# Attention with top-k, then two feed-forward blocks: a step's order remade on four engines

## The reference

```python
scores = scale * np.matmul(q, k.transpose(0, 1, 3, 2))
kth = np.partition(scores, -top_k, axis=-1)[..., -top_k:-top_k + 1]
scores = np.where(scores >= kth, scores, -1000000000.0)
attn = np.exp(scores - np.max(scores, axis=-1, keepdims=True))
x = heads_side_by_side(np.matmul(attn / (attn.sum(-1, keepdims=True) + 1e-09), v))
h = x @ w_in
g = np.maximum(h, 0.0) + alpha * np.minimum(h, 0.0)
y = g @ w_out
out = (y @ w_a) * (y @ w_b) @ w_o
```

## Time and profile before

| | |
|---|---|
| median of 3 runs | 655.65 us (655.42 to 656.97) |
| profiled execution | 659.29 us, of it the span 657.5 us |
| PE busy | 607.9 us, 92% |
| VectorE (DVE) busy | 425.1 us, 65% |
| ScalarE (ACT) busy | 355.5 us, 54% |
| GpSimd (POOL) busy | 291.3 us, 44% |
| busy tenths of VectorE in 40 slices | 4999999999899999999999006364331222112111 |
| busy tenths of PE in 40 slices | 5577799998999999899898989989999999999997 |

### The profile page before, as it was taken

How to read it: one execution, slowest core, us unless ns; L and a number is a source line. 1 busy time by engine, 2 the same in 40 slices (tenths; PEclk the granted TensorE clock), 3 DMA queues, 4 the chain that set the end, 5 groups by cost and what they waited for, 6 DMA issues and landing times.

```text
span 657.5 us, 10894 instructions
## 1 busy us (share of the span) xinstructions
PE 607.9 (92%) x4192; PEld 507.8 (77%) x4192; DVE 425.1 (65%) x847; ACT 355.5 (54%) x642; POOL 291.3 (44%) x285
## 2 busy tenths in 40 slices
PE   5577799998999999899898989989999999999997
PEld 3355576676787878777776867879999999999996
DVE  4999999999899999999999006364331222112111
ACT  3499987877777777776667536353322122121111
POOL 0266779899988898877878650000000000000000
PEclk9889989999999999999999989989999999999999
DMA  7889962223113333342240430840011000010001
GB/s 258 318 295 368 353 224 62 78 67 85 58 42 96 125 110 106 103 129 93 79 127 21 157 121 17 283 164 1 0 49 49 0 1 1 0 49 1 0 1 48
DMA packets 30914, 68.06 MB, mean 104 GB/s; under 512 B 2704, under 2 KB 7312, under 8 KB 30736
## 3 DMA queue, kind: packets, MB, share of 16 engines
q1 hardware_dynamic: 30864, 67.38, 30.9%
HBM read 53.22 MB, written 14.16 MB: 102 GB/s over the span
## 4 chain that ended last, share of the span: by engine, by line
PE 50%; DVE 34%; POOL 8%; issue 4%; ACT 2%; DMA 2%; SPq 0%; ACTq 0%; POOLq 0%
DVE top L700 18%; DVE work L708 16%; PE ps L962 7%; PE ps L960 7%; PE ps L961 7%; PE ps L974 4%; PE ps L975 4%; PE ps L973 4%; PE ps L860 2%; PE ps L862 2%; PE ps L861 2%; POOL p_sb L432 2%; POOL wout_lo L419 2%; PE ps L892 2%; PE ps L895 2%
## 5 line engine op out<-in xcount | busy, mean ns | idle before, releaser
L700 DVE MAX8 top<-work 128x8 f32<-128x576 f32 x216 | 152.4, 749 | 0.0
L432 POOL TENSOR_TENSOR p_sb<-s_sb,p_sb 128x576 f32<-128x576 f32 x72 | 101.8, 1426 | 18.6 <-ACT p_sb L534 18.6
L708 DVE MATCH_REPLACE8 work<-top,work 128x576 f32<-128x576 f32 x144 | 106.1, 746 | 0.0
L753 DVE TENSOR_TENSOR ab<-ps,a_sb 128x384 f32<-128x384 f32 x36 | 20.1, 558 | 132.3 <-PE ps L962 132.3
L960 PE MATMUL ps<-y_parts,wab 128*128 128x384 f32 x288 | 97.3, 338 | 0.0
L962 PE MATMUL ps<-y_parts,wab 128*128 128x384 f32 x288 | 96.7, 336 | 0.0
L961 PE MATMUL ps<-y_parts,wab 128*128 128x384 f32 x288 | 96.4, 335 | 0.0
L540 ACT ACTIVATE p_sb<-p_sb,neg_max 128x576 f32<-128x576 f32 x72 | 56.4, 784 | 50.0 <-POOL p_sb L432 49.9
L860 PE MATMUL ps<-win_hi,xT_parts 128*128 128x512 f32 x144 | 61.2, 425 | 11.1 <-POOL xT_parts L449 8.4
L534 ACT ACTIVATE p_sb<-s_sb,kth_big 128x576 f32<-128x576 f32 x72 | 55.3, 787 | 11.0 <-POOL neg_max L427 11.0
L669 ACT ACTIVATE ab_hi<-ab 128x384 fp32r<-128x384 f32 x36 | 18.9, 524 | 77.2 <-DVE ab L753 77.2
(11 more groups left out here) (88 smaller groups left out, 1350.5 us busy)
## 6 DMA issues: line engine op xcount, KB each, us to landing
v_sb<-in_v SPq DMA_DIRECT2D x36, 320.0 KB, 2.9
s_dram<-keep_sb SPq DMA_DIRECT2D x16, 576.0 KB, 4.8
s_sb<-s_dram SPq DMA_DIRECT2D x16, 576.0 KB, 3.7
k_sb<-in_kT SPq DMA_DIRECT2D x24, 288.0 KB, 4.1
win_raw<-in_w_in SPq DMA_DIRECT2D x4, 1024.0 KB, 7.4
wout_raw<-in_w_out SPq DMA_DIRECT2D x4, 1024.0 KB, 9.0
wab_raw<-in_w_a SPq DMA_DIRECT2D x8, 384.0 KB, 3.9
...
```

The costliest lines, as they stand in the source:

```text
L432: nc.gpsimd.tensor_tensor(p_sb[:, chain.par, c, :], s_sb[:, chain.slot, c, :], p_sb[:, chain.par, c, :], ALU.subtract).then_inc(masked, 1)
L700: largest = nc.vector.max(top32[:, pair.par, c, 8 * r:8 * r + 8], work[:, c, :] if r else s_sb[:, pair.slot, c, :])
L708: nc.vector.match_replace(work[:, c, :], top32[:, pair.par, c, 8 * r:8 * r + 8], work[:, c, :] if r else s_sb[:, pair.slot, c, :], -3.0e38)\
```

## The change

A pair is turned and multiplied by v one step earlier: the first part of pair i + 1 is turned in the step in which it is masked, `times_v` of pair i runs in step i. The x turn and the first block follow one step earlier (FIRST_UP 4, last step 35). h itself is turned (`copy_of_h`, `turn_h`), and max(h, 0), max(-h, 0), slope and sum come after the turn, with features along partitions: alpha is then one column per 128 features, loaded as 8 KB in place of 1 MB, and the transposed result needs one more step to its high part (`hi_of_g`). The keys of batch 0 are loaded once into SBUF. The split tile is the second, not the first. Four slots, not two, hold kept scores; they lie where w_out is loaded later. The first scores wait for the query and half the keys, and are made head by head. The orders of all four engines within a step, and in the tail, are rewritten. The rest of the tail goes on in the pattern shown.

```diff
-SLOTS = 2
+SLOTS = 4
 FIRST_STEP = -2
-LAST_STEP = N_PAIRS
-FIRST_UP = PAIRS + 1
+LAST_STEP = N_PAIRS - 1
+FIRST_UP = 4
 LAST_UP = LAST_STEP - FIRST_UP
-AHEAD = {-2: [0, 1, 2], -1: [3, 4, 5], 0: [6, 7], 1: [8, 9], 2: [10, 11], 3: [12, 13], 4: [14, 15]}
-W_IN_AT = {-1: [0], 0: [1], 1: [2], 2: [3], 3: [4], 4: [5], 5: [6], 6: [7]}
+AHEAD = {-2: [0, 1], -1: [2, 3, 4], 0: [5, 6, 7], 1: [8, 9, 10], 2: [11, 12, 13], 3: [14, 15]}
+W_IN_AT = {-1: [0], 0: [1], 1: [2], 2: [3], 3: [4, 5], 4: [6], 5: [7]}
 W_OUT_AT = {7: [0], 8: [1], 9: [2, 3], 10: [4], 11: [5, 6], 12: [7]}
-LOADS_AT = {-1: ["in1"], 0: ["in2"], 1: ["in3"], 2: ["out0"], 3: ["out1"], 4: ["alpha", "out2"], 5: ["out3"]}
+LOADS_AT = {-2: ["in0"], -1: ["in1"], 0: ["in2"], 1: ["alpha", "in3"], 4: ["out0"], 5: ["out1"], 6: ["out2"], 7: ["out3"]}
+DVE_FROM = LAST_UP - 1
+SPLIT = 1
...
+        keep_sb = at("keep_sb", [P, SLOTS, 2 * S], reg_wout_lo)
+        qa_sb = at("qa_sb", [P, KEPT // PAIRS, PAIRS, P], reg_wout_lo + 4 * SLOTS * 2 * S)
+
+        k_sb, reg_att = new("k_sb", [P, PAIRS, S])
         q_sb, _ = new("q_sb", [P, KV, P])
...
         def x_turn(i):
 
-            tile, rest = divmod(i - FIRST_UP, QUADS)
-            return tile if rest == 0 and 0 <= tile and i <= LAST_STEP else None
+            tile, rest = divmod(i - PAIRS + 1, PAIRS)
+            return tile if rest == 0 and 0 <= tile < TILES else None
...
-            for p in range(KV):
-                load_kq(pair(p))
-                load_k1(p)
-            load_qa(WHOLE + 1)
-            for p in range(KV, PAIRS):
-                load_k1(p)
-            load_first_block("in0")
+            load_q(pair(0))
+            sp.dma_start(k_sb[0:D, 0, :], kT[0, 0, 0:D]).then_inc(k0_half_in, 16)
+            sp.dma_start(k_sb[D:P, 0, :], kT[0, 0, D:P]).then_inc(k0_in[0], 16)
+            load_q(pair(1))
+            load_k0(1)
+            load_qa(0)
+            load_k1(0)
+            load_k1(1)
+            load_k0(2)
+            load_k1(2)
+            load_k0(3)
+            load_k1(3)
+            load_qa(1)
             for p in range(2):
                 sp.wait_ge(scored, p + 1)
-                load_kq(pair(KV + p))
-            load_qa(WHOLE + 2)
-            for i in range(FIRST_STEP, LAST_STEP):
+                load_q(pair(KV + p))
+            for i in range(FIRST_STEP, LAST_STEP + 1):
                 if i == FIRST_STEP + 1:
                     load_v(pair(0))
                     load_v(pair(1))
...
                 if i > FIRST_STEP and i + 5 < DIRECT:
                     sp.wait_ge(scored, i + 4)
-                    load_kq(pair(i + 5))
-                if i in (0, 1):
-                    sp.wait_ge(ahead, PAIRS * (i + 1))
-                    load_qa(WHOLE + 3 + i)
+                    load_q(pair(i + 5))
+                if i in (-1, 0):
+                    load_qa(i + 3)
                 for n in AHEAD.get(i, []):
                     save_scores(n)
+                if i == min(n for n in LOADS_AT if LOADS_AT[n][0] == "out0"):
+                    for slot in range(SLOTS):
+                        sp.wait_ge(kept_saved[slot], 16 * KEPT // SLOTS)
...
             def slope_and_sum(seq):
                 q = seq % QUADS
-                pool.wait_ge(u_free, up_use(seq) + 1)
-                nc.gpsimd.tensor_tensor(neg[:, :], neg[:, :], alpha_sb[:, q * 512:(q + 1) * 512], ALU.mult)\
-                  .then_inc(slope_done, 1)
+                pool.wait_ge(halves_done, seq + 1)
+                if 0 < seq < QUADS + 1:
+                    pool.wait_ge(down_done, seq)
+                sides = neg[:, :].rearrange("p (f n) -> p f n", f=QUADS)
+                slopes = alpha_sb[:, q * QUADS:(q + 1) * QUADS].unsqueeze(2).to_broadcast([P, QUADS, P])
+                nc.gpsimd.tensor_tensor(sides, sides, slopes, ALU.mult).then_inc(slope_done, 1)
                 pool.wait_ge(slope_done, seq + 1)
-                nc.gpsimd.tensor_tensor(pos[:, :], pos[:, :], neg[:, :], ALU.subtract).then_inc(sum_done, 1)
+                if seq > QUADS:
+                    pool.wait_ge(ghi_done, seq - QUADS)
+                nc.gpsimd.tensor_tensor(gT[:, :, :].rearrange("p f n -> p (f n)"), pos[:, :], neg[:, :], ALU.subtract)\
+                  .then_inc(sum_done, 1)
 
             def lo_of_g(seq):
-                pool.wait_ge(ghi_done, seq + 1)
+                pool.wait_ge(ghi_done, seq + 1 - QUADS)
                 nc.gpsimd.tensor_tensor(g_lo, gT[:, :, :], g_hi.bitcast(f32), ALU.subtract).then_inc(glo_done, 1)
 
             def step(i):
-                chain, output, finished = pair(i + 1), pair(i), pair(i - 1)
+                chain, output = pair(i + 1), pair(i)
                 if chain is not None:
                     bound(chain)
+                if x_turn(i - 1) is not None:
+                    lo_of_x(x_turn(i - 1))
                 if output is not None and output.hp == PAIRS - 1:
                     denominator(output)
-                if turning(i) is not None:
-                    slope_and_sum(turning(i))
+                if rounded(i) is not None and QUADS <= rounded(i) < DVE_FROM:
+                    lo_of_g(rounded(i))
                 if chain is not None:
                     mask(chain, 0)
-                if x_turn(i) is not None:
-                    lo_of_x(x_turn(i))
-                if finished is not None and finished.hp == PAIRS - 1:
-                    normalise(finished)
-                if chain is not None:
-                    mask(chain, 1)
                 for c in W_IN_AT.get(i - 1, []):
                     lo_of_w_in(c)
                 for c in W_OUT_AT.get(i - 1, []):
                     lo_of_w_out(c)
-                if turning(i) is not None and turning(i) >= QUADS:
-                    lo_of_g(turning(i))
+                if chain is not None:
+                    mask(chain, 1)
+                if output is not None and output.hp == PAIRS - 1:
+                    normalise(output)
+                if turning(i) is not None and turning(i) < DVE_FROM:
+                    slope_and_sum(turning(i))
 
             for i in range(FIRST_STEP, LAST_STEP + 1):
                 if i == FIRST_UP + 1:
                     pool.wait_ge(alpha_in, 16)
                 step(i)
-            slope_and_sum(LAST_UP)
...
+                if c == 0:
+                    act.wait_ge(pv_done, (SPLIT + 1) * PAIRS)
+                    act.wait_ge(kept, KEPT)
...
-                at = SC[0] + c * S
-                act.wait_ge(scored, 1)
+                at = SC[1 - c] + c * S
+                if c == 0:
+                    act.wait_ge(half_scored, 1)
+                else:
...
-            def halves_of_h(seq):
+            def copy_of_h(seq):
                 act.wait_ge(u_full, up_use(seq) + 1)
                 if seq:
                     act.wait_ge(gt_full, seq)
-                else:
-                    for slot in range(SLOTS):
-                        act.wait_ge(kept_saved[slot], 16 * KEPT // SLOTS)
-                nc.scalar.activation(pos[:, :], ps[:, U, :], ACT.Relu)
-                nc.scalar.activation(neg[:, :], ps[:, U, :], ACT.Relu, scale=-1.0).then_inc(u_free, 1)
-
-            def parts_of_g(seq):
-                src = ps[:, GT, :].rearrange("p (f n) -> p f n", f=QUADS)
+                nc.scalar.activation(h_sb[:, :], ps[:, U, :], ACT.Copy).then_inc(u_free, 1)
+
+            def halves_of_h(seq):
                 act.wait_ge(gt_full, seq + 1)
                 if seq:
+                    act.wait_ge(sum_done, seq)
+                nc.scalar.activation(pos[:, :], ps[:, GT, :], ACT.Relu)
+                nc.scalar.activation(neg[:, :], ps[:, GT, :], ACT.Relu, scale=-1.0).then_inc(halves_done, 1)
+
+            def hi_of_g(seq):
+                act.wait_ge(sum_done, seq + 1)
+                if seq > QUADS:
                     act.wait_ge(down_done, seq)
-                if seq < QUADS:
-                    nc.scalar.activation(gT[:, :, :], src, ACT.Copy).then_inc(ghi_done, 1)
-                else:
-                    nc.scalar.activation(g_hi, src, ACT.Copy)
-                    nc.scalar.activation(gT[:, :, :], src, ACT.Copy).then_inc(ghi_done, 1)
+                nc.scalar.activation(g_hi, gT[:, :, :], ACT.Copy).then_inc(ghi_done, 1)
...
-                score, chain, output, finished = direct(i), pair(i + 1), pair(i), pair(i - 1)
+                score, chain, output = direct(i), pair(i + 1), pair(i)
                 ahead_now = AHEAD.get(i, [])
-                if turning(i) is not None:
-                    halves_of_h(turning(i))
-                if output is not None:
-                    evict_turned(output, 0)
+                if x_turn(i - 1) is not None:
+                    evict_x_turn(x_turn(i - 1))
+                if rounded(i) is not None and rounded(i) >= QUADS:
+                    hi_of_g(rounded(i))
                 if chain is not None:
                     relu(chain, 0)
-                if x_turn(i) is not None:
```

(114 more changed lines are left out.)

136 lines of the change are left out of this document (87 added, 49 removed).

## The result

The changed kernel takes 660.4 us in the median (659.65 to 665.5) against 655.5 for the kernel before on the same chip: ratio 1.0087, 95% interval 1.0064 to 1.0111. It is 4.8 us slower, where 4.5 us faster was forecast, and lies above the range.

What follows compares the result with a forecast made beforehand. VectorE's ranking at 9.66 us a pair, then PE's tail, bound the kernel. Span 657.5 - 1.1 (start) + 3.8 (middle) - 7.2 (tail) = 653.0; the change of -4.5 put on the median 655.65 gave 651.2 us, range 644.5 to 656.5.

Steps and rivals of the forecast that it cites:

- the edits costed at nothing: Side edits priced at nothing, among them four keep slots, alpha's load, k loads and ScalarE's work per quad.
- The walk through the middle: Ranking from step 6: GpSimd's same-step waits for down and heavy steps make VectorE wait 6.95 against 3.14, 3.8 us lost.
- Start: First scores, made head by head after smaller loads, let VectorE start ranking earlier: gain 1.1 us (0.3 to 1.9).
- Slope: GpSimd's slope with alpha as a broadcast operand takes 1046 ns, not 1289: 0.24 us off each quad.
- Tail: End of ranking to second block: 52.4 us against 60.3, 7.9 shorter, of which 7.2 was counted.
- The two waits of 1.6: Tail: PE idles 1.6 us before down(32) and again before down(33), as one up does not hide a quad's chain.
- (d): Rival: waits for lo_of_x at each tile's first up bring PE to 1.2 GHz, 2.3 us each, five times: 662.7; chance 0.10.
- (b): Rival: the middle is worse, slope at 1289 (+1.2) and a wait before up(4) slowing PE (+2.3): 654.7; chance 0.09.
- (c): Rival: the tail's two waits of 1.6 us slow PE's clock, some 1.5 us each: 654.2; chance 0.05.

Runs made afterwards that it cites:

- g2: e8 with saved scores spread 4, 3, 3, 2, 2, 2 and, in steps with two saves, both through the second score buffer; 657.7 us.
- e2: Changed kernel with a second place for g, so GpSimd's slope_and_sum in steps 7 to 9 waits for the down of the step before; 661.0 us.
- g1: Changed kernel with w_out's parts in earlier steps: two each in steps 7 and 8, then one a step; 656.4 us.
- g6: Kernel before the change with w_out's parts in steps 7: 0 and 1, 8: 2 and 3, then one a step; 653.4 us.
- e7: Changed kernel with w_a and w_b parts moved behind copy_of_h in the tail, lo_of_w2 behind lo_of_g, tile 7's y evicted earlier; 660.7 us.
- e6: Changed kernel with the second turn of a pair ahead of the direct score in PE's step, in all steps; 666.2 us.
- e8: Changed kernel with the second turn ahead of the direct score in steps -2 to 3 only; 658.7 us.
- e10: Changed kernel with GpSimd's low parts of w_in and w_out behind the second mask of the step, not between the masks; 664.3 us.
- e1: Changed kernel with the 16 saved scores spread 4, 3, 3, 2, 2, 2 over steps -2 to 3 in place of 2, 3, 3, 3, 3, 2; 666.4 us.
- e13: Changed kernel with work left out: GpSimd makes w_out's low part for 64 of 512 columns, PE uses the high part instead; 657.3 us.
- e3: Changed kernel with VectorE's reciprocal in the last of the four rounds instead of the second; 664.7 us.
- e4: Changed kernel with the edits of e1, e2 and e3 together; 665.9 us.
- b0: A second profiled execution of the kernel before, with no edit; 656.18 us.
- b5: Kernel before with only the change's spread of saved scores, 2, 3, 3, 3, 3, 2 in steps -2 to 3; 658.7 us.

## Why the prediction was wrong

**The step that failed** is the sentence on four keep slots under the edits costed at nothing: "Three scores ahead in a step instead of two make ScalarE's early steps about 9.9 us against 9.66, and the copy has more than 6 us to spare." It counted ScalarE's busy time and put the effect at nothing. What sets the early step is a ring over two engines: ScalarE's saved copy at the end of its step, PE's direct score that needs its buffer, PE's turn behind the score, ScalarE's copy of the turned pair, relu, and the next copies. ScalarE's copies of pairs 5, 6 and 7 and PE's wait before the first x turn in the changed kernel:

```profile
52.49 1.12 ACT L537 ACTIVATE s_sb<-ps 128x1152 f32<-128x1152 f32 x1
...
62.71 1.12 ACT L537 ACTIVATE s_sb<-ps 128x1152 f32<-128x1152 f32 x1
...
76.05 1.12 ACT L537 ACTIVATE s_sb<-ps 128x1152 f32<-128x1152 f32 x1
```

```profile
70.17 0.44 PE L916 MATMUL ps<-ident,x_sb 128*128 128x128 f32 x1 [3.86 <-ACT keep_sb L554]
```

A step takes 10.2 us at best in this ring, and the one with the first x turn 13.3 (76.05 - 62.71): `turn_x(0)` waits for the last save, the score of pair 7 stands behind it, and PE runs at a granted 0.50 from 70 to 75. Of the room of 6.7 us 2.7 were left before the heavy steps began, and pair 7 waited 2.38 us besides. g2 takes the ring away and the copy comes at 79.9: ranking ends 4.3 us earlier, at 365.9. The step with the first x turn stays 13.4 us long even there (copies at 58.40 and 71.75), with the same wait for the last save; no run takes that wait away. The span missed its forecast by 8.1 us (3.6 slower for 4.5 faster), and 4.3 of them are this ring.

**The walk through the middle** had the right increments on a wrong start. GpSimd's timeline of the changed kernel, two slopes of the light steps and then the bounds of steps 10 to 13:

```profile
99.01 1.04 POOL L476 TENSOR_TENSOR neg<-neg,alpha_sb 128x512 f32<-128x512 f32 x1 [2.11 <-PE ps L957]
...
122.82 1.04 POOL L476 TENSOR_TENSOR neg<-neg,alpha_sb 128x512 f32<-128x512 f32 x1 [3.47 <-PE ps L957]
...
136.35 0.19 POOL L442 TENSOR_SCALAR kth_big<-top 128x2 f32<-128x2 f32 x1
...
148.23 0.19 POOL L442 TENSOR_SCALAR kth_big<-top 128x2 f32<-128x2 f32 x1
...
158.88 0.19 POOL L442 TENSOR_SCALAR kth_big<-top 128x2 f32<-128x2 f32 x1
...
171.75 0.19 POOL L442 TENSOR_SCALAR kth_big<-top 128x2 f32<-128x2 f32 x1
```

The steps from 136.35 take 11.9, 10.7 and 12.9 us; 11.6, 10.6 and 12.8 were forecast. But the first is at 136.35, forecast 129.9, and all are 6.4 to 6.9 late. With the ring open (g2) it is at 132.12, so the ring makes 4.2 us of that, and 2.2 are the walk's own error, in the steps before; which of its terms is open. VectorE still waits 10.2 us in g2, where 6.95 were forecast. The waits for `down` in steps 6 to 9 came as foretold, 2.11, 1.44, 3.47 and 2.12. They cost 2.5 us (e2). Two parts of w_out in one GpSimd step cost 4.5 (g1), but most of this is not what the change added: the kernel before paid 3.2 us for them by its median, 2.4 by VectorE's waits (g6). The forecast named GpSimd's heavy steps but did not ask whether they could be moved.

**Start.** Right, and a little more: first score at 4.2 as said, ranking from 7.18, 1.7 to 1.8 us gained, 1.1 forecast.

**Slope.** GpSimd took 1.04 us with the broadcast operand, as taken from the normalisation, not 1.29. The Trainium skill ("GPSIMD Engine Reference", section 3.1), by which the repeated operand would save nothing, is contradicted by the trace for a second instruction.

**Tail.** 55.0 for a forecast of 52.4, both from E, the end of ranking. PE ended up(33) at E + 28.7, as forecast. Then PE's timeline, which answers to the earlier trace rows:

```profile
401.18 0.47 PE L960 MATMUL ps<-wout_hi,g_parts 128*128 128x512 f32 x1 [2.31 <-ACT ytok L619]
...
408.70 0.50 PE L960 MATMUL ps<-wout_hi,g_parts 128*128 128x512 f32 x1 [1.35 <-DVE g_parts L782]
...
416.71 0.55 PE L940 MATMUL ps<-ident,h_sb 128*128 128x128 f32 x3 [1.76 <-ACT h_sb L598]
...
422.29 0.50 PE L960 MATMUL ps<-wout_hi,g_parts 128*128 128x512 f32 x1 [0.85 <-DVE g_parts L782]
...
425.16 0.33 PE L1027 MATMUL ps<-y_parts,wab 128*128 128x384 f32 x1
```

The two waits of 1.6 are there, as 2.31 and 1.35. The first waits for tile 7's y, which ScalarE evicts behind two parts of w_a and the copy of h(33); the last copy of h waits behind a part of w_a too (1.76, forecast 0.8); and the 0.85 before down(35), the same chain once more, was left out of the sum. e7 moves these parts and gets 1.9 us back.

The tails of 55.0 to 58.1 fall into groups by what the profiles show. It is 55.0 (after, e6) where the granted clock stayed at 1.00 from the tile's last first `up`, 17 us before E, on, and 55.5 in e8. It is 56.0 to 56.1 (g1, g2, e10) where the clock fell behind that `up`'s wait of 2.2 us. A fall behind the wait of 2.31 ahead of down(32) adds 1.5 us to either, 56.6 (e1) and 57.5 (e2, e13). It is 58.0 and 58.1 with the late reciprocal of e3 and e4. The tail of before holds such a fall too: granted 0.57 from 389 to 393 in b0, tail 60.3; without it, in b5, the same tail is 58.7. Like against like the change makes the tail 3.7 us shorter, and some 1.5 us of the 60.3 that the forecast started from were the clock's.

**Rivals.** (d) has the nearest number, 662.7, and is near by luck. Its event came: PE waits 2.2 us for lo_of_x before the first up of steps 20, 24, 28 and 32 (1.55 were taken), and behind two of these waits the clock fell. PE's timeline and a stretch of the changed kernel, in the form of the earlier trace rows:

```profile
314.30 0.77 PE L929 MATMUL ps<-win_hi,xT_parts 128*128 128x512 f32 x1 [2.20 <-POOL xT_parts L466]
```

```profile
314.00:318.00 4.00, 3.70 (x10) 2.97 (x11) 4.00 (x10) 1.84 (x4) 4.00 (x4) 0.57 0.00 0
```

Its cost did not: VectorE waits for nothing after 205.86, and a fall just ahead of the tail is worth 1.0 us there (56.0 against 55.0), not 2.3. The loss lies before 205.86, where the waits for lo_of_x are 1.49 (114.36) and 1.04 (160.71) and the granted clock is 1.00 from 86 to 205. (b)'s slow up(4) did not come. (c) did not in the changed kernel's profile, where the clock was 1.00 through the tail, but it did in three others with the same tail (e1, e2, e13), at the 1.5 us that it named. The clock fell in the early steps too, which no rival named.

**What stays open.** Why the medians of e1, e3 and e10 lie 4 to 6 us above the changed kernel: e3's long tail makes 3 us of its 4.3, but that the edits themselves slow PE's clock early on was not tried. And what in the walk puts GpSimd 2.2 us late at step 10 without the ring.
